# Attention, MLP and experts on one core: a shorter bias table, sums shared by two engines, first MLP products inside the last head pair

## The reference

```python
# attention, q k v (2, 8, 768, 64), n_global 8, n_local 96
scores = matmul(q, k.T) / 8
is_global = key < n_global
is_local  = (rel >= 0) & (rel < n_local)        # rel = query - key
dist   = where(is_global & ~is_local, n_local, |rel|)
scores = where(is_global | is_local, scores - slope[h] * dist, -1e9)
a = exp(scores - max(scores)); a = a / (sum(a) + 1e-9)
x = (a @ v) laid out as (1536 tokens, 512)
# MLP, w_in (512, 2048), w_out (2048, 512)
h = x @ w_in
x = (h * tanh(log1p(exp(h)))) @ w_out
# experts, w1 (4, 512, 1024), w2 (4, 1024, 512)
y = sum_e p[:, e] / (sum(p) + 1e-9) * (relu(x @ w1[e]) @ w2[e])
```

## Time and profile before

| what | value |
|---|---|
| median of 3 runs | 916.49 us (912.8 to 917.21) |
| the profiled execution: device time | 915.88 us |
| its span, from first to last instruction | 913.8 us |
| mean granted clock of TensorE, share of full speed | 0.983 |
| busy: TensorE | 873.1 us (96% of the span) |
| busy: VectorE | 506.8 us (55%) |
| busy: ScalarE | 315.7 us (35%) |
| busy: GpSimd | 266.0 us (29%) |
| chain that ended last: TensorE 69%, VectorE 21%, ScalarE 7% | |

### The profile page before, as it was taken

How to read it: one execution, slowest core, us unless ns; L and a number is a source line. 1 busy time by engine, 2 the same in 40 slices (tenths; PEclk the granted TensorE clock), 3 DMA queues, 4 the chain that set the end, 5 groups by cost and what they waited for, 6 DMA issues and landing times.

```text
span 913.8 us, 12568 instructions
## 1 busy us (share of the span) xinstructions
PE 873.1 (96%) x4884; PEld 441.3 (48%) x4884; DVE 506.8 (55%) x1016; ACT 315.7 (35%) x591; POOL 266.0 (29%) x218
## 2 busy tenths in 40 slices
PE   3878998999999999999999999999999999999998
PEld 3766786444444444444444444444444444444443
DVE  7855876999999999996642225322134322212121
ACT  3699885545454555454030111101020101101020
POOL 1266994122222232320009500059000193000000
PEclk8798999999999999999999999999999999999999
DMA  9762340000000000202000400000400000000001
GB/s 220 242 220 55 82 156 1 1 1 1 0 1 10 1 0 1 78 18 93 4 6 0 151 34 0 7 1 2 182 1 0 6 0 0 1 24 23 34 12 49
DMA packets 52005, 39.20 MB, mean 43 GB/s; under 512 B 40816, under 2 KB 41712, under 8 KB 51440
## 3 DMA queue, kind: packets, MB, share of 16 engines
q1 hardware_dynamic: 49888, 34.31, 12.5%
q10 hardware_dynamic: 2064, 4.19, 1.3%
HBM read 35.35 MB, written 3.15 MB: 42 GB/s over the span
## 4 chain that ended last, share of the span: by engine, by line
PE 69%; DVE 21%; ACT 7%; issue 2%; DMA 0%; POOL 0%; DVEq 0%; SPq 0%; ACTq 0%
PE bank L635 58%; PE bank L658 5%; DVE tmp L1299 4%; DVE tmp L1317 3%; PE bank L540 2%; DVE xT L1315 2%; DVE tmp L1297 2%; PE bank L566 2%; DVE tmp L1303 2%; ACT scaled L841 2%; PE bank L585 1%; DVE hid L1309 1%; ACT tmp L824 1%; ACT tmp L858 1%; ACT tmp L953 1%
## 5 line engine op out<-in xcount | busy, mean ns | idle before, releaser
L927 ACT ACTIVATE hid<-bank 128x512 f16<-128x512 f32 x96 | 57.3, 596 | 410.6 <-PE bank L635 410.6
L635 PE MATMUL bank<-xT,wA 128*128 128x512 f16 (+1 forms) x864 | 196.2, 381 | 1.1 <-DVE acc L1114 1.1
L1290 DVE SCALAR_TENSOR_TENSOR hid<-bank,hid 128x512 f16<-128x512 f32 x96 | 66.4, 692 | 172.3 <-ACT hid L927 172.3
L658 PE MATMUL bank<-hid,wB 128*128 128x512 f16 x576 | 132.2, 379 | 4.4 <-ACT acc L911 2.6
L635 PEld LDWEIGHTS bank<-xT,wA 128*128 128x128 f16 x864 | 84.8, 98 | 103.7 <-issue 2.2
L790 POOL TENSOR_TENSOR tmp<-tmp 128x512 f32<-128x512 f32 x48 | 70.1, 1460 | 198.2 <-DVE tmp L1317 198.2
L635 PE MATMUL bank<-wA,hid 128*128 128x512 f16 x576 | 125.3, 379 | 0.0
L635 PE MATMUL bank<-xT,wB 128*128 x576 | 125.3, 379 | 0.0
L635 PE MATMUL bank<-wB,hid 128*128 128x512 f16 x576 | 125.3, 379 | 0.0
L745 POOL TENSOR_SCALAR stage<-stage,sc 128x1024 f32<-128x1024 f32 x32 | 35.9, 1120 | 252.8 <-DVEq L1283 240.8
L1366 DVE SCALAR_TENSOR_TENSOR acc<-bank,pg,acc 128x512 f32<-128x512 f32 x36 | 27.0, 751 | 131.7 <-PE bank L635 131.7
(11 more groups left out here) (110 smaller groups left out, 930.6 us busy)
## 6 DMA issues: line engine op xcount, KB each, us to landing
stage<-in_moe_w SPq DMA_DIRECT2D x8, 2048.0 KB, 9.1
stage<-in_moe_w_in SPq DMA_DIRECT2D x1, 4096.0 KB, 14.2
wB<-in_moe_w_out ACTq DMA_DIRECT2D x1, 4096.0 KB, 15.9
hid<-in_q SPq DMA_DIRECT2D x16, 192.0 KB, 3.2
hid<-in_k SPq DMA_DIRECT2D x16, 192.0 KB, 3.4
xT<-in_v SPq DMA_DIRECT2D x8, 384.0 KB, 5.1
out_y<-acc SPq DMA_DIRECT2D x12, 256.0 KB, 2.0
rows<-max SPq DMA_DIRECT2D x4, 128.0 KB, 4.2
```

The costliest lines, as they stand in the source:

```text
L635: last = pe.matmul(dst, lhs(c, a), rhs(c, b), start=(c == 0 and n == 0), stop=(c == chunks - 1 and n == 2))
L658: last = pe.matmul(psum(4 + d), w_out_s[:, a, f // 2, f % 2, d * P:(d + 1) * P], hv[:, T % RING, b, :], start=(f == 0 and n == 0), stop=(f ...
L927: act.activation(hv[:, f, 0, :], psum(f % 4), ACT.Relu).then_inc(f_hi, 1)
L1290: dve.scalar_tensor_tensor(hv[:, f, 1, :], psum(f % 4), 0.0, hv[:, f, 0, :], ALU.max, ALU.subtract).then_inc(f_ready, 1)
```

## The change

Five things are changed.

1. *The start of attention.* The key and distance tables are now made of four VectorE instructions instead of eight (`band_tables`); one that needs no bounds and the three fills with zero are done before the bounds arrive. The fills of pair 0 go q0, k0, q1, k1 into four banks of their own, and the first scores wait for the first two. TensorE does 13 matmuls of 128x128 on the identity (`keep_busy`) ahead of the first fill and 3 behind the scores of unit 2. `biased` of unit 2 and the maximum of v piece 1 move ahead of the wait for the scale of v and of the low half of v piece 0. ScalarE sums |v| of pieces 3, 5 and 7 (`values_sum`); VectorE keeps 0, 1, 2, 4 and 6.
2. *`FILL`*: q0, k0, q1, k1 in all pairs instead of q0, q1, k0, k1.
3. *|w_in| and |w_out|*: ScalarE sums pieces 0, 2, 4, 6 in units 21, 23, 25, 27 (and 33 to 39), VectorE takes the maximum of |w| in pieces 1, 3, 5, 7 in units 22 to 28 (and 34 to 40).
4. *First products early* (`EARLY`): those of T = 0 and the first half of T = 1 are issued in the last three units of the last pair, six matmuls in each, between the turn of unit u and the product with v of unit u - 2.
5. *`TURN_AT`*: x of group 1 is turned behind T = 1 and x of group 2 behind T = 3.

The diff, cut to its core:

```diff
-        TURN_AT = {0: 1, 2: 2}
+        TURN_AT = {1: 1, 3: 2}
+
+        EARLY = [(0, (0, 1)), (0, (2, 3)), (1, (0, 1))]
...
+        V_SUMS = list(range(3, PAIRS, 2))
...
-        FILL = [(j, t) for j in range(2) for t in (range(HEAD), range(HEAD, QT))]
+        FILL = [(j, t) for t in (range(HEAD), range(HEAD, QT)) for j in range(2)]
...
-                    last = pe.transpose(psum(k if m_0 else 3, P, n * P), nat[slot][j][:, t * P:(t + 1) * P], ident[:])
+                    last = pe.transpose(psum(4 + k if m_0 else 3, P, n * P), nat[slot][j][:, t * P:(t + 1) * P], ident[:])
...
-                if u == 0:
-
+                if banded and before(i, slot) is None:
+                    if u in (0, 2 * HEAD):
+                        pe.wait_ge(tr_out, 2 if u == 0 else FILLS)
+                elif u == 0:
                     pe.wait_ge(tr_out, FILLS * (2 * i + slot + 1))
...
+            def keep_busy(times):
+
+                for _ in range(times):
+                    pe.matmul(psum(3, P), ident[:], ident[:], start=True, stop=True)
+
...
+                        if not after(i, slot) and u >= UNITS - len(EARLY):
+                            n = u - (UNITS - len(EARLY))
+                            if n == 0:
+                                pe.wait_ge(x_ready, DC)
+                                pe.wait_ge(w_split, 1)
+                            first_product(*EARLY[n])
                         if behind:
                             pv(*behind, banded)
...
                 for T in range(STEPS + LAG):
-                    if T < STEPS:
+                    if banded and T < 2:
+                        if T:
+                            first_product(1, (2, 3))
+                    elif T < STEPS:
                         first_product(T)
...
                     if T in TURN_AT:
+                        pe.wait_ge(o_ready, 2 * PAIRS + 2)
                         pe.wait_ge(x_ready, DC * TURN_AT[T])
...
             pe.wait_ge(ident_ready, 1)
+            keep_busy(13)
...
-                if n + c:
-                    act.wait_ge(w_piece, PIECES * n + c)
+                act.wait_ge(w_sum, PIECES // 2 * n + c // 2 + len(V_SUMS))
...
-                        if start <= at < start + PIECES:
+                        if at - start in range(0, PIECES, 2):
...
+                    if at + 1 in V_SUMS:
+                        values_sum(at + 1)
...
+            dve.wait_ge(iotas, 3)
+            dve.scalar_tensor_tensor(rel_b, rel_b, -1.0e9, rel_b, ALU.mult, ALU.max)
+            for s in s_b:
+                last = dve.memset(s[:, 2 * P + GLOBAL_COLS:3 * P], 0.0)
+            link(last)
+
             dve.wait_ge(bounds_in, 32)
...
-                dve.tensor_reduce(wpieces[:, c:c + 1], stage[:, at:at + PIECE], AX_X, ALU.max,
+                src = w_out_raw if n == 1 else stage
+                dve.tensor_reduce(wpieces[:, c:c + 1], src[:, at:at + PIECE], AX_X, ALU.max,
...
+                    if first is not None and at - first in range(1, PIECES, 2):
+                        weights_part(n, at - first)
...
-                    elif ahead:
+                    elif ahead and ahead != (0, 0, 2):
                         biased(*ahead, banded)
...
+                if is_banded:
+                    biased(0, 0, 2, is_banded)
                 dve.wait_ge(v_amax, 1)
                 make_scale(chain(scale_step), scale_cols(SC_V0))
                 dve.sem_inc(v_scale, 1)
+                value_step(0)
                 values_low(0)
-                pair(0, 0, is_banded, value_step)
+                pair(0, 0, is_banded, lambda u: u and value_step(u))
```

More of the change, by code:

```diff
@@ L176, in program @@
         W = 3 * P
-        dist_b, key_b, loc_b = (scratch(BAND_COLS) for _ in range(3))
+        dist_b, key_b = (scratch(BAND_COLS) for _ in range(2))
         s_b = [scratch(W) for _ in range(3)]
@@ L396, in run_attention @@
                 run(True)
-                rest()
+                rest(True)
             with eng.Else():
                 run(False)
-                rest()
+                rest(False)
         block = ctx.enter_context(nc.Block())
@@ L587, in pv, with split_product, first_product @@
                 last.then_inc(pv_done, 1)
+            def split_product(dst, lhs, rhs, chunks, fresh=None, only=None):
+                for c in only or range(chunks):
+                    if fresh is not None:
+                        fresh(c)
+                    for n, (a, b) in enumerate(((0, 0), (0, 1), (1, 0))):
+                        last = pe.matmul(dst, lhs(c, a), rhs(c, b), start=(c == 0 and n == 0),
+                                         stop=(c == chunks - 1 and n == 2))
+                return last
+            def first_product(T, only=None):
+                g, f = divmod(T, FT)
+                if T >= 4:
+                    pe.wait_ge(b_ready, T - 3)
+                last = split_product(psum(T % 4), lambda c, s: w_in_s[:, s, c, f * P:(f + 1) * P],
+                                     lambda c, s: xs(g, c, s), DC, only=only)
+                if not only or DC - 1 in only:
+                    last.then_inc(h_psum, 1)
             def pair(i, slot, banded):
@@ L623, in pair, with rest @@
                     share_max(1)
[L625 to L645, removed]
+            def rest(banded):
                 def second_product(T):
@@ L883, in pair @@
                     act.wait_ge(w_max, 1)
-                    for c in range(PIECES):
+                    for c in range(0, PIECES, 2):
                         weights_sum(1, c)
@@ L1134, in matrix_step @@
                 for n, col in ((0, SC_WIN), (1, SC_WOUT)):
+                    first = W_SUMS[case].get(n)
+                    if first is not None and at - first in range(1, PIECES, 2):
+                        weights_part(n, at - first)
                     if at == W_MAX[case].get(n):
@@ L1150, in value_step @@
             def value_step(u):
-                if u + 1 < PAIRS:
-                    n = u + 1
+                n = u + 1
+                if n < PAIRS and n not in V_SUMS:
                     dve.wait_ge(v_loaded[n], 16)
@@ L1378, in _ @@
             with dve.If(banded == 1):
-                link = chain(table_step)
-                dve.wait_ge(iotas, 3)
-                band_tables(link)
+                band_tables(chain(table_step))
                 dve.wait_ge(band_ready, 1)
-                for s in s_b:
-                    last = dve.memset(s[:, 2 * P + GLOBAL_COLS:3 * P], 0.0)
-                link(last)
                 attention(True)
@@ L1392, in _ @@
                 dve.sem_inc(tables_free, 1)
+                for c in range(1, PIECES, 2):
+                    weights_part(1, c)
                 weights_max(1)
```

44 lines of the change are left out of this document (29 added, 15 removed).

## The result

The changed kernel took 918.49 us (median of 15 runs, 916.97 to 922.33), the kernel before beside it 915.96 us (15 runs). The ratio is 1.0035, with a 95% interval of 1.0022 to 1.0047: slower by 2.5 us, where 920.3 was forecast. The profiled execution has a span of 915.1 us against 913.8. One execution of the kernel before, beside e5 to e8, took 5127 us; the ratios leave it out.

A forecast was written before the change was run, and what follows sets the result against it. TensorE was taken as the bound from the second product 0 on, and before it mostly a VectorE-ScalarE chain. 915.88 − 4.5 + 0 + 4.5 + 3.8 = 919.7, plus 0.6 for the median: 920.3 us, range 908 to 924.5.

The forecast's parts named there:

- The start: Start of attention to the end of v's reads: shorter table and moved reads give −4.5 us, bounds −6 and −3.
- the matmuls on the identity: TensorE's first work: the 13 matmuls end before q and k have landed and cost nothing there.
- The order of the fills: Fills in attention: each stays in its unit and all are wanted only by the next pair, 0 us.
- The sums of |w|: Alternate units in attention: ScalarE's sum and VectorE's reduce don't overlap; stretches 16.77 and 17.95 us, +4.5 us in all.
- The early products: Last pair of attention: some of the moved 3.9 us hides, so VectorE's first tile starts 1.8 us sooner.
- The later turn of x: Before the second product 0: VectorE needs 18.44 us from its first tile, so that product starts 1.9 us later.
- the clock: At the second product 0: 6.5 us of TensorE idle time brings half clock, costing 2.4 us.
- wait for L911: TensorE's 2.6 us of waits behind ScalarE: 0.5 us may go, 2.2 stays.
- parts 4 and 5: Early products and later turn of x together: +1.9 + 2.4 − 0.5 = +3.8 us, bounds −2 and +5.
- A: Rival on the sums of |w|: both engines' sums run side by side, −7 instead of +4.5, 908.8 us; chance 0.14.
- B: Rival on the early products: they pay in full, 3.9 us, no lower clock; 911.6 us; chance 0.13.
- C: Rival on the start: its gain is not there, −1 instead of −4.5, 923.8 us; chance 0.16.

The follow-up runs named there:

- e5: Changed kernel with reduces of |w| in units of ScalarE's sums, ScalarE's |v| sums in units of VectorE's reads, x turned behind T = 0 and 1: 905.27 us.
- e8: Changed kernel with all sums of |w| on ScalarE, no early first products and the old turns of x: 908.64 us, ratio 0.9930 against before.
- e3: Changed kernel with all sums of |w_in| and |w_out| on ScalarE again: 911.68 us, ratio 0.9969 against before.
- e4: Changed kernel with VectorE's reduces of |w| moved into the same units as ScalarE's sums: 909.83 us, ratio 0.9937 against before.
- e2: Changed kernel without the early first products and with the old turns of x: 914.02 us, ratio 0.9988 against before.
- e10: e6 without the early first products: 903.04 us (4 runs), ratio 0.9863 against before.
- e9: e8 with TensorE's wait for o_ready back ahead of the first product of T = 0: 909.85 us, ratio 0.9945 against before.
- e7: Changed kernel without the 13 and the 3 matmuls on the identity: 919.46 us, ratio 1.0044 against before.
- e11: The changed kernel itself measured again: 918.57 us, ratio 1.0040 against before.
- e1: Changed kernel with x of groups 1 and 2 turned behind T = 0 and T = 2 again, early products kept: 915.17 us, ratio 0.9998 against before.
- e6: e5 with 12 more matmuls on the identity where TensorE waits for the scale of v: 904.27 us, ratio 0.9879 against before.

## Why the prediction was right, and where a step was off

The forecast was 920.3 us, 3.8 slower than the median known then; measured were 2.5 slower. Step by step:

- *The start*, −4.5: the table and the moved reads measured −4.4 at the end of v's reads. The first `biased` came at 11.48, not at 10.9. The step that failed is that the matmuls on the identity end before q and k land and cost nothing: they delayed the fills by 1.3 us, which the faster transposes gave back. The sum held since the read of piece 1 and `biased` of unit 2 were worth 1.7 us (2.4 to 4.1) instead of 1.3.
- *The order of the fills*, 0: no run changed it alone.
- *The sums of |w|*, +4.5: 16.81 us by the table where the chain gave 16.77, and 18.01 where it gave 17.95. This chain, followed from row to row, was the best number of the forecast. e3 and e4 show its reason from both sides.
- *The early products*: VectorE's first tile was 7.1 us behind exp 96 instead of 9.3, 2.2 sooner (1.8 forecast). But I gave this to the early products. Without them, and with the wait for o_ready moved, it is 6.4 us (e2, e8, e10); with that wait in its old place it is 9.3 (e9). So the 2.2 us are 2.9 from the moved wait, with the half clock that went along, less 0.7 for the early products. The step that failed is the term of the early products, −1.8, which should have been +0.6 to +0.7; a line that I had not priced made up for it, and that the number came near is luck. I wrote of the half clock over T = 0, and not of the wait ahead of it.
- *The later turn of x*: 18.40 us from the first tile to the second product 0, 18.44 forecast; idle time 6.35 us, 6.5 forecast; the clock 2.5 us, 2.4 forecast. The reason that I gave for the clock was misread, though. The two rows of lower clock don't stand behind longer idle time than 1.75 us: TensorE had been idle for 1.39 us ahead of the one at 34.20 and for 1.08 ahead of the one at 154.00, and a wait of 2.15 us at 340 was followed by 1.00. So before, the trace did not bear out that long gaps bring the lower clock and short ones keep it; that 6.3 us did so is shown by the changed kernel, e3, e4, e7 and e11. Of the wait for L911 (L944 in the changed kernel) 1.1 us went and not 0.5: this term was mis-sized.
- *The sum*: parts 4 and 5 are +1.4 at the second product 0 relative to exp 96, +2.5 for the clock, −1.1 for the wait: +2.8 instead of +3.8. With −4.4 for the start and +4.6 for the sums that is +3.0 in all. The remaining difference to the 1.3 us of the two spans is pair 1, where the profiled execution of before lost 1.5 us to the clock and that of the changed kernel did not. The medians differ by 2.5; that this loss evens out over many executions would fit, but no run shows it.

Of the rivals, A (side by side) is excluded for the change as it was written, but it is just what e4 makes of it. B falls by e1, e2 and e10; its own sum was also uneven, 911.6 in one place and 911.8 in the other, and only the second follows from its terms. C falls by e8.

## What to carry to other kernels

Where two engines hand work to each other in every unit, splitting extra work between them pays only if both halves stand in the same unit: in alternate units the two add up in one chain, and 8 pieces on one engine were faster than 4 and 4 (911.68 and 918.49 us). Moving work of an engine that isn't the bound at that place (here 18 matmuls) brings nothing. A step put later so that TensorE stands idle for 6.35 us, as the turn of x here, is paid twice, once as idle time and once in TensorE's clock. A wait that stands earlier than it must can cost more than its own length for the same reason: in the traces 1.1 us of waiting cost 2.9, of which the medians show 1.2.

## What the runs showed of the hardware

- The same program keeps or loses the upper clock behind the same gap from one execution to the next: 1.4 us of idle time, then 1.00 in one profile and 0.53 in another, for 1.5 us of time. Likewise 1.1 us of idle time behind the last product with v was followed by half clock in before and e9, and not in e1, e5 and e6, where early products stand ahead of it; and 2.92 us ahead of the second product 0 in e1 was not followed by it. The length of the last gap alone doesn't tell.
- The 13 matmuls of 128x128 on the identity, first work of TensorE, took 4.6 us in one execution (e8) and 5.7 in another (changed kernel): the spacing of their records halved at 6.4 us in the one and not before their end in the other.
- A read of 128x1024 on VectorE and one on ScalarE that overlap (e4) took 1.21 and 1.05 us, against 1.21 and 1.04 alone.

What stays open is what decides between the two levels behind a short gap, and whether the hold of e6 settles pair 1; the runs don't separate e5, e6 and e10 from each other beyond their spread.
